# A half query tile's maximum product moved into the score phase of a fused attention kernel, as two row halves

## The reference

```
q_pool = q.reshape(B, H, S // 2, 2, D).mean(axis=3)        # B 4, H 8, S 1152, D 64
scores = scale * np.matmul(q_pool, k.transpose(0, 1, 3, 2))
scores = scores - np.max(scores, axis=-1, keepdims=True)
attn = np.exp(scores)
attn = attn / (np.sum(attn, axis=-1, keepdims=True) + 1e-09)
out = np.matmul(attn, v)
```

## Time and profile before

| | us |
|---|---|
| median of 3 executions | 734.81 |
| lowest and highest | 733.58, 735.74 |
| profiled execution | 734.46 |
| its span | 732.7 |
| granted TensorE clock, mean over the span | 0.988 of full |

### The profile page before, as it was taken

One profiled execution on the slowest core, in us unless ns is written; L12 is line 12 of the kernel. 1 busy time (PEld: TensorE's weight loads), 2 busy tenths in 40 slices (PEclk: granted clock), 3 DMA queues, 4 the chain that ended last, 5 costly groups with the idle time before them and its releaser, 6 DMA issues.

```text
span 732.7 us, 17254 instructions
## 1 busy us (share of the span) xinstructions
PE 718.9 (98%) x6343; PEld 552.1 (75%) x6343; DVE 514.5 (70%) x1015; ACT 466.6 (64%) x1072; POOL 486.9 (66%) x431
## 2 busy tenths in 40 slices
PE   7999999999999999999999999999999999999997
PEld 5787787787877878778787777434778888888886
DVE  6788888888888888888888847434895545555542
ACT  3678788787887878878778763215655454545453
POOL 2479889898898898988989871213774444444442
PEclk8799999999999999999999999999999999999999
DMA  5032423425334243342443338899201010101011
GB/s 146 27 77 65 137 95 114 151 90 163 102 99 166 89 156 109 98 166 89 133 132 99 105 126 294 303 387 387 101 1 44 1 43 1 43 0 43 0 44 43
DMA packets 51626, 81.86 MB, mean 112 GB/s; under 512 B 14556, under 2 KB 20572, under 8 KB 51548
## 3 DMA queue, kind: packets, MB, share of 16 engines
q1 hardware_dynamic: 51180, 80.37, 34.5%
q10 hardware_dynamic: 368, 0.46, 0.2%
HBM read 75.94 MB, written 4.79 MB: 110 GB/s over the span
## 4 chain that ended last, share of the span: by engine, by line
PE 92%; DVE 3%; POOL 2%; issue 2%; ACT 1%; DMA 0%; SPq 0%; DVEq 0%; POOLq 0%; ACTq 0%
PE ps L704 19%; PE ps L1017 8%; PE ps L1018 8%; PE ps L1016 8%; PE ps L685 6%; PE ps L687 6%; PE ps L689 5%; PE ps L683 5%; PE ps L651 4%; PE ps L715 3%; PE ps L596 3%; PE ps L647 2%; PE ps L1006 2%; PE ps L930 2%; PE ps L900 2%; PE ps L638 2%
## 5 line engine op out<-in xcount | busy, mean ns | idle before, releaser
L1103 ACT ACTIVATE probs<-ps 128x576 f32<-128x576 f32 x288 | 181.4, 652 | 26.7 <-PE ps L689 22.2
L564 POOL TENSOR_TENSOR g_lo<-g_buf,g_hi 128x384 fp32r<-128x384 f32 x96 | 101.9, 1064 | 101.0 <-ACT g_hi L1283 101.0
L1414 DVE TENSOR_REDUCE mx<-ps 128x1 f32<-128x512 f32 x248 | 161.8, 684 | 3.3 <-PE ps L651 1.6
L704 PE MATMUL ps<-probs,v_sb 128*64 128x288 f32 x1152 | 146.8, 409 | 0.0
L527 POOL TENSOR_TENSOR p_sum<-p_sum,probs 128x576 f32<-128x576 f32 x93 | 144.7, 1582 | 0.0
L683 PE MATMUL ps<-q_hi,k_hi 64*128 64x288 f32 x576 | 126.4, 302 | 1.0 <-ACT q_neg L1142 1.0
L685 PE MATMUL ps<-q_hi,k_lo 64*128 64x288 f32 x576 | 123.3, 295 | 0.0
L687 PE MATMUL ps<-q_lo,k_hi 64*128 64x288 f32 x576 | 123.0, 294 | 0.0
L689 PE MATMUL ps<-q_neg,k_one 64*128 64x288 f32 x576 | 122.8, 293 | 0.0
L704 PEld LDWEIGHTS ps<-probs,v_sb 128*64 128x64 f32 x1152 | 79.5, 137 | 56.4 <-issue 5.2
L1660 DVE SCALAR_TENSOR_TENSOR v_buf<-u_buf 128x384 f32<-128x384 f32 x96 | 60.2, 627 | 86.9 <-ACT u_buf L1276 86.2
(11 more groups left out here) (230 smaller groups left out, 1315.9 us busy)
## 6 DMA issues: line engine op xcount, KB each, us to landing
pre<-in_moe_w SPq DMA_DIRECT2D x41, 512.0 KB, 4.5
v_sb<-in_v SPq DMA_DIRECT2D x32, 288.0 KB, 3.4
k_raw<-in_k SPq DMA_DIRECT2D x31, 288.0 KB, 3.7
q_raw<-in_q SPq DMA_DIRECT2D x32, 256.0 KB, 3.9
from_x<-in_moe_w SPq DMA_DIRECT2D x9, 512.0 KB, 4.5
p_inv<-inv_dram SPq DMA_DIRECT2D x62, 72.0 KB, 2.6
out<-o_stage SPq DMA_DIRECT2D x34, 128.0 KB, 2.4
staged<-in_moe_w SPq DMA_DIRECT2D x8, 512.0 KB, 5.2
```

The lines of the kernel that those rows point to most:

```text
L704: mm = pe.matmul(ps[D * h:D * h + D, 4, 0:HALF], v_sb[n % 2][:, u, :], probs[:, u, HALF * h:HALF * h + HALF], start=(i == 0), stop=(i == N ...
L1103: nc.scalar.activation(dst, ps[:, b0:b0 + 2, 0:HALF], ACT.Exp, scale=SCORE_SCALE).then_inc(exp_done, 1)
L1414: top = nc.vector.tensor_reduce(mx[:, NC * t + g:NC * t + g + 1], ps[:, b, :], AX.X, ALU.max)
```

## The change

The product of the half query tile is made in the score phase of the head before it, as two products of 64 rows that accumulate in one bank (first g = 0, then g = 1). The bank is 5, the second of the pair that step 2 uses. The second half waits for max_full, which shows that the first half and the ends of g = 1 are complete. The ends change places: g = 1 comes first, into bank 7, and g = 0 second, into bank 6. Steps 0 and 2 of the scores are cut in two: in step 0 the first rest half and the ends of g = 1 come ahead, the second rest half and the ends of g = 0 between parts 1 and 2; in step 2 the row product comes between parts 1 and 2. Step 2 now also waits for the reduction of the half tile. From step 3 on a row product stands ahead of each step as before, under a number lower by two.

On VectorE the order in tops is: ends of g = 1, half tile, ends of g = 0, eight rows; the reciprocal follows the fifth row. Nothing of the maxima is left behind weigh.

```
--- before.py
+++ after.py
@@ -215,13 +215,16 @@
             return 2 if j % 2 == 0 else 4
 
         def unit_bank(u):
-            return 6 + u % 2
+            return 7 - u % 2
 
         def rest_bank(m):
-            return job_bank(QT) if m == 0 else 7
+            return job_bank(QT) if m == 0 else 5
 
         def units_of(m):
             return JOBS + UNITS * (m - 1) if m > 0 else 0
+
+        def products_of(m):
+            return JOBS + (UNITS + 1) * (m - 1) if m > 0 else 0
 
         def step_bank(n, s):
             if s % 3 == 2:
@@ -627,30 +630,33 @@
                                        k_hi[0][rows_of(g), 0:KP], start=True, stop=True)
                 mm.then_inc(max_full, 1)
 
-            def row_max_rest(m):
-                if m == 0:
-                    pe.wait_ge(max_free, QT - 1)
-                elif m == 1:
+            def row_max_rest_first():
+                pe.wait_ge(max_free, QT - 1)
+                pe.matmul(ps[:, rest_bank(0), :], q_rest[0][:, :], k_hi[0][:, 0:KP], start=True, stop=True).then_inc(max_full, 1)
+
+            def row_max_rest(m, g):
+                if g == 0:
+                    pe.wait_ge(rounded, ROUNDS * (m + 1))
+                else:
+                    pe.wait_ge(max_full, products_of(m) + 2)
+                pe.matmul(ps[:, rest_bank(m), :], q_rest[m % 2][rows_of(g), :], k_hi[m % 2][rows_of(g), 0:KP],
+                          start=(g == 0), stop=(g == 1)).then_inc(max_full, 1)
+
+            def row_max_ends(m, g):
+                if m == 1:
                     pe.wait_ge(turn_free, 4)
                 else:
-                    pe.wait_ge(rounded, ROUNDS * (m + 1))
                     pe.wait_ge(max_free, units_of(m))
-                pe.matmul(ps[:, rest_bank(m), :], q_rest[m % 2][:, :], k_hi[m % 2][:, 0:KP],
+                for i, t in enumerate((0, 1) if g == 0 else (2, 3, QF)):
+                    mm = pe.matmul(ps[:, 6 + g, P * i:P * i + P], q_hi[m % 2][rows_of(g), P * t:P * t + P],
+                                   k_hi[m % 2][rows_of(g), KP:KP + P], start=True, stop=True)
+                mm.then_inc(max_full, 1)
+
+            def row_max(m, u):
+                pe.wait_ge(max_free, units_of(m) + (1 if u == 0 else u + 2))
+                t, g = u // 2, u % 2
+                pe.matmul(ps[:, unit_bank(u), :], q_hi[m % 2][rows_of(g), P * t:P * t + P], k_hi[m % 2][rows_of(g), 0:KP],
                           start=True, stop=True).then_inc(max_full, 1)
-
-            def row_max(m, u):
-
-                pe.wait_ge(max_free, units_of(m) + u)
-                b, g = unit_bank(u), u % 2
-                if u < 2:
-                    for i, t in enumerate((0, 1) if g == 0 else (2, 3, QF)):
-                        mm = pe.matmul(ps[:, b, P * i:P * i + P], q_hi[m % 2][rows_of(g), P * t:P * t + P],
-                                       k_hi[m % 2][rows_of(g), KP:KP + P], start=True, stop=True)
-                else:
-                    t = u // 2 - 1
-                    mm = pe.matmul(ps[:, b, :], q_hi[m % 2][rows_of(g), P * t:P * t + P], k_hi[m % 2][rows_of(g), 0:KP],
-                                   start=True, stop=True)
-                mm.then_inc(max_full, 1)
 
             def turn_neg_max(m):
                 pe.wait_ge(neg_max_ready, m + 1)
@@ -659,20 +665,23 @@
                     pe.wait_ge(exp_done, NT * (m - 1) + NT - 1)
                 pe.transpose(ps[:, neg_bank(m), 0:P], neg_max[:, :], ident[:]).then_inc(neg_full, 1)
 
-            def scores(n, s, halves):
-
-                if s == 0:
-                    pe.wait_ge(neg_free, n + 1)
-                    if n == 0:
-                        pe.wait_ge(turn_free, 3)
-                if s == 1 and 0 < n < HEADS - 1:
-                    pe.wait_ge(turn_free, 2 * n + 4)
-                if s == 2 and 0 < n < HEADS - 1:
-                    pe.wait_ge(x_read, n)
-                if s >= 3:
-                    pe.wait_ge(exp_done, NT * n + s - 2)
+            def scores(n, s, halves, parts=range(4)):
+
+                if parts[0] == 0:
+                    if s == 0:
+                        pe.wait_ge(neg_free, n + 1)
+                        if n == 0:
+                            pe.wait_ge(turn_free, 3)
+                    if s == 1 and 0 < n < HEADS - 1:
+                        pe.wait_ge(turn_free, 2 * n + 4)
+                    if s == 2 and n < HEADS - 1:
+                        pe.wait_ge(max_free, units_of(n + 1) + 2)
+                        if n > 0:
+                            pe.wait_ge(x_read, n)
+                    if s >= 3:
+                        pe.wait_ge(exp_done, NT * n + s - 2)
                 b0 = step_bank(n, s)
-                for part in range(4):
+                for part in parts:
                     for g in halves:
                         rows = rows_of(g)
                         h = g if s == 0 else (s - 1) % 2
@@ -687,7 +696,8 @@
                             mm = pe.matmul(out, k_hi[n % 2][rows, t], q_lo[n % 2][rows, cols], start=False, stop=False)
                         else:
                             mm = pe.matmul(out, k_one[rows, :], q_neg[n % 2][rows, cols], start=False, stop=True)
-                mm.then_inc(scores_ready, 1)
+                if parts[-1] == 3:
+                    mm.then_inc(scores_ready, 1)
 
             def weigh(n):
 
@@ -763,25 +773,50 @@
             row_max_first(3)
             turn(1, 1)
             row_max_first(4)
-            row_max_rest(0)
+            row_max_rest_first()
             pe.wait_ge(max_free, QF + 1)
             warm(6, 2)
             turn_neg_max(0)
             warm(5, 5)
             pe.wait_ge(consts_ready, 1)
             pe.wait_ge(zeroed, 1)
+            def scores_with_maxima(n, s):
+                if s == 0:
+                    if n > 0:
+                        row_max_rest(n + 1, 0)
+                        row_max_ends(n + 1, 1)
+                        scores(n, s, (0, 1), (0, 1))
+                        row_max_rest(n + 1, 1)
+                        row_max_ends(n + 1, 0)
+                        scores(n, s, (0, 1), (2, 3))
+                    else:
+                        scores(n, s, (0, 1))
+                        row_max_rest(1, 0)
+                        row_max_ends(1, 1)
+                elif s == 1:
+                    if n == 0:
+                        scores(n, s, (0, 1), (0, 1))
+                        row_max_rest(1, 1)
+                        row_max_ends(1, 0)
+                        scores(n, s, (0, 1), (2, 3))
+                        row_max(1, 0)
+                    else:
+                        row_max(n + 1, 0)
+                        scores(n, s, (1, 0))
+                elif s == 2:
+                    scores(n, s, (0, 1), (0, 1))
+                    row_max(n + 1, 1)
+                    scores(n, s, (0, 1), (2, 3))
+                else:
+                    row_max(n + 1, s - 1)
+                    scores(n, s, (1, 0) if s % 2 == 1 else (0, 1))
+
             for n in range(HEADS):
                 for s in range(NT):
-                    if 0 < n < HEADS - 1 and s == 0:
-                        row_max(n + 1, 0)
-                        row_max(n + 1, 1)
-                    if n + 1 < HEADS and s > 0:
-                        row_max(n + 1, s + 1)
-                    scores(n, s, (1, 0) if s % 2 == 1 and n + 1 < HEADS else (0, 1))
-                    if n == 0 and s == 0:
-                        row_max_rest(1)
-                        row_max(1, 0)
-                        row_max(1, 1)
+                    if n + 1 < HEADS:
+                        scores_with_maxima(n, s)
+                    else:
+                        scores(n, s, (0, 1))
                     if n == HEADS - 1 and s == 3:
                         pe.wait_ge(phi_loaded, 16)
                         logits(0, range(0, KD // 2))
@@ -793,8 +828,6 @@
                 if n + 1 < HEADS:
                     turn_neg_max(n + 1)
                 weigh(n)
-                if n + 2 < HEADS:
-                    row_max_rest(n + 2)
                 add_up(n)
 
 
@@ -1396,23 +1429,25 @@
                 top.then_inc(max_free, 1)
 
             def top_of_rest(m):
-                dve.wait_ge(max_full, JOBS if m == 0 else units_of(m) + 1)
+                dve.wait_ge(max_full, JOBS if m == 0 else products_of(m) + 3)
                 nc.vector.tensor_reduce(mx[:, QF * NC:QF * NC + 1], ps[:, rest_bank(m), :], AX.X, ALU.max).then_inc(max_free, 1)
 
+            def top_of_ends(m, g):
+                b = 6 + g
+                dve.wait_ge(max_full, products_of(m) + (2 if g == 1 else 4))
+                top = nc.vector.tensor_reduce(
+                    mx[:, 2 * NC * g:2 * NC * g + 2 * NC].rearrange("p (i c) -> p i c", c=NC)[:, :, NC - 1],
+                    ps[:, b, 0:2 * P].rearrange("p (i k) -> p i k", i=2), AX.X, ALU.max)
+                if g == 1:
```

(30 more changed lines are left out.)

## The result

The changed kernel takes 743.96 us (median of 4, 742.67 to 744.86), the kernel before 734.21 in the same comparison: ratio 1.0128, 95% interval 1.0103 to 1.0153. That is +9.75 us where +13.5 was forecast; direction and range held. The profiled execution took 742.67 us, its span is 740.9.

A forecast was written before the change was run, and what follows sets the result against it. It took GpSimd's loop, without slack, to bound the kernel at 13.17 us a head. The third step's +0.45 gave 13.62, above 13.47 through VectorE and TensorE; over 30 heads +13.5, so 748.0, range 743.5 to 751.5.

The forecast's parts named there:

- the GpSimd loop: Per head, GpSimd's additions, ones product, score phase to its third step, exponential: 3.42 + 8.95 + 0.17 + 0.63 = 13.17 us, the whole period.
- No slack: Claim that GpSimd's line fills the whole 13.17 us period, TensorE waiting for its last addition ahead of the ones product.
- rival B: Faster: removing the product between weigh and ones product gives 0.43, the phase takes 0.21; -6.6 us, 728; chance 0.07.
- The third step: Third step of scores (s = 2) in a head's score phase: end moves from 2.65 to about 3.1 after phase start, +0.45.
- P0: Moment a head's score phase begins, its first weight load (208.81 in the kernel before); times in us count from it.
- mid step 2: Maximum product in the middle of score step 2: needs the ends of half 0 reduced, load forecast at P0 + 2.32.
- The phase's end: End of a head's score phase: row products wait for VectorE's reductions, the last at 6.2 instead of 5.48, +0.73.
- the other loop: Loop through VectorE and TensorE, per head: 13.17 + 0.73 - 0.43 = 13.47 us.
- rival A: Slower by less: VectorE keeps up, third step moves 0.2 to 0.28, period 13.4, +7.5, 742 us; chance 0.20 together with E.
- alone worth nothing: Removing the half tile's product between weigh and ones product (at most 0.43) gains nothing alone, since GpSimd covers it.
- the third reduction: VectorE's reduction of the rest, now in line from P0: three reductions ahead of step 2's product where two were.
- the added columns: 512 more columns on each half of the array's rows in the score phase: some 0.23, 0.2 at the least.

## Why the prediction was right, and where it was not

*The bound.* "The whole period is the GpSimd loop" became true with the change; the run with the shorter addition shows it (8.6 us back, where the same cut gave 1.2 in the kernel before). "No slack" was wrong: 0.12. The release from GpSimd takes 0.05 (209.23 to 209.28), not the 0.17 that the earlier trace rows shows for GpSimd's own next instruction; before, the exit of the 128-row product held the ones product. The rival B had that doubt, and was right in its reason for 0.12 and not for its 0.43.

*The third step, forecast +0.45.* Measured 212.60 + 0.29 = 212.89, P0 + 2.98, +0.33. The forecast walked one load slot of 0.11 too far: loads on different halves of the array need not queue (two stand at 209.91), so VectorE began at P0 + 0.59 and not 0.70, and all that waited for it came 0.1 sooner: row product of step 1 at 1.26 (forecast 1.36), mid step 2 at 2.22 (2.32). The waits themselves were the ones named, each 0.04 to 0.06 behind its reduction.

*The term that was missing.* GpSimd's second addition starts 1.54 behind the first, before it followed without a gap (1.39 behind the first's start); the whole line was 8.95. It needs the exponential of step 4, which ends at 214.48 + 0.65 = 215.13 in the kernel after:

```profile
214.48 1.25 ACT L1136 ACTIVATE probs<-ps 128x576 f32<-128x576 f32 x2
```

GpSimd follows at 215.21. VectorE's late line reaches GpSimd a second time here, +0.13. This and the slack of 0.12 cancelled, so the sum was off by the 0.1 of the third step alone. That was luck: the prediction had neither.

*The phase's end, forecast +0.73:* 7.05 against 6.46, +0.59, the same slot. It gave 13.33 for the other loop (forecast 13.47), as measured by the run with the shorter addition.

*The number.* 743.96 lies at the lower edge of the forecast's own range (743.5) and nearer to rival A's 742 than to 748.0. A's mechanism (the third step later by 0.2 to 0.28, with VectorE keeping up) was not what happened: 0.33, with a wait for VectorE at each row product.

*The signs.* The period, the third step's end and the last row product (load at P0 + 6.08, named 6.2) came as said. GpSimd's wait ahead of its first addition grew by 0.2 and not by half a microsecond, because the rest of the longer period went into its line of additions. VectorE's idle piece was 1.33 and not 1.8: of its 1.9 idle in a head before, 1.1 stand at two other waits, for the rounded queries (9.5 us in 23 heads) and for the transposed maxima (16.5 in 22), and these two stayed (11.2 and 16.5 in 22 after).

*The removal "alone worth nothing":* wrong. 7.6 us, of which the slack is about half; the rest goes with the ends of g = 1, which no longer wait for the bank that the half tile shared with them.

*The cause.* The prediction put the shift down to the third reduction and the added columns. The reduction is shown (0.16 of the period's 0.36, 6.3 us by the medians). But the order that came with it is at least as large: alone it costs 11.5 us over the kernel before (14 over the kernel with the same bank), and the moved product then costs nothing more, because it gives its 0.43 back. These are not parts of one sum: with the whole change GpSimd's loop holds, with the order alone TensorE's and VectorE's. How the cost divides between the cut of step 0 and the exchange of the ends was not tried.

## What to carry to other kernels

Where one engine (here VectorE) is only just in time to read what a fully busy one (TensorE) writes, list for each product which reduction frees its bank. The order of the small groups at the start of a phase was worth more here (11.5 us) than the product that was to be moved (7.6), and the banks of these groups and of the half tile were worth 5.2. The engine that the profile names for a wait need not be what sets it: before the change it named GpSimd, which was done 0.12 us early. Take the named engine's work away in an experiment before calling it the bound. Price a removal by leaving the work out, before moving it.

## What was not expected of the hardware

A 128-row product between products of another shape took 0.43 us from load to load wherever it stood: behind weigh (207.75 to 208.18; 206.28 to 206.71 with GpSimd early) and at P0 (201.08 to 201.51), while 512 columns add only some 0.23 to a half of the array (the prediction's estimate from 0.10 for 224 columns).

Weight loads for the two halves of the array can start at the same time (209.91 twice), where the first three of the kernel before, two of one half and one of the other that waited for its bank, stand some 0.11 apart.
